# Where GpSimd waits for its scatters in a mixture-of-experts loop, and how its loop is closed

## The chip, the cores and the metric

The kernel runs on one core of a Trainium2 chip. The metric is the device time of one execution in microseconds (us): the median of the runs.

## The reference

A batch of 4 sequences of 768 tokens goes through a linear attention with decay (8 heads of 48), a dense layer pair 384 to 2048 to 384 with a leaky ReLU, and last a gated layer of 8 experts of which each token takes at most one. Only the last part bears on the change:

```
do_compute = x @ w_skip > 0
xc = x[do_compute]
logits = xc @ w_gate
e_idx = np.argmax(logits, axis=1)
for e in range(E):
    mask = e_idx == e
    h = np.maximum(xc[mask] @ w1[e], 0.0)
    y[mask] = gate_w[mask, None] * (h @ w2[e])
out[do_compute] = xc + y
```

The inputs are float32 and the result is a table of 3072 rows of 384 values.

## The kernel before

Attention and the dense layers are computed in eight groups of three chunks of 128 tokens. Each finished row z goes to DRAM twice, to a table `z_rows` and to `out`, while the routing of each chunk writes lists of token numbers by expert (`scatter`, line 1869). The expert part then works in blocks of up to 128 tokens of one expert. Two blocks of the busiest expert are done ahead of a loop, written out in full (names with `_a`, `AHEAD = 2`). All others are done in a loop over blocks whose number, `blocks`, is known only at run time (a value read from `plan`, at most 31). Each engine runs its own copy of the loop, `Fori(0, 8)` with four blocks written out in its body (`UNROLL = 4`) and an `If` on every turn and on every block. Every matmul is three products of high and low parts.

For block j of the loop:
- GpSimd (POOL) has gathered the block's rows of `z_rows` into `zg[u]`, u = j mod 4, with an indirect DMA (`gather`, line 1928).
- TensorE turns them (line 887), multiplies by w1 (line 964), turns the hidden rows (line 986) and multiplies by w2 into one of two banks (line 1003). ScalarE and VectorE make the high and low parts of what comes between (lines 1292 and 1820 for the hidden rows), and those of the next expert's weights.
- VectorE writes `res[j mod 2]` as bank times gate plus `zg[u]` (line 1844). It waits first for the product, `s_ey_done`, and for `s_res_free >= j + 1` (line 1843), which says that the buffer's last scatter has landed.
- GpSimd scatters `res[j mod 2]` to `out` with an indirect DMA (line 1962). Each such DMA adds 16 to `s_rows_out` when it has landed.

GpSimd's program around the loop sets the order of this. Before the loop it adds 1 to `s_res_free` (line 1935), gathers blocks 0 to 3 and scatters the two blocks done ahead (`scatter_ahead`, line 1903), which also count on `s_rows_out`. In `put_rows(j, ...)` it waits until all scatters before block j, those two included, have landed (line 1951) and adds 1 to `s_res_free`; copies the block's ids to `put` (line 1953); if there is a block j + 4, waits for the gather of block j and copies ids to `get` (line 1926); waits for `res` of block j; scatters it; and gathers block j + 4.

Its loop is in two levels: `part` of 0 and 1 (line 1970), each with an `If` whether that half has any block (line 1971), and in it four turns `jj` (line 1972) with an `If` of their own (line 1973). The other engines have one level of eight turns (VectorE: lines 1810 and 1811). After the loop GpSimd waits for all scatters (line 1978); then the block of engine programs closes with a branch, a DRAIN and a barrier on each engine (shown under line 100).

Of the kernel before, what the change touches and what calls it, by code (L numbers as in the profile page):

```python
# [42 lines left out]
TOKENS = B * S  # L43
# [4 lines left out]
BLOCKS = 31  # L48
# [4 lines left out]
UNROLL = 4  # L53
# [7 lines left out]
AHEAD = 2  # L61
# [31 lines left out]
def build(nc, rk_t, rk_nat, v_nat, w_cols, u_rows, win, wout, wout_t, gates, experts, consts, out, z_rows):  # L93
# [6 lines left out]
    with ctx:  # L100
# [3 lines left out]
        def sem(name):  # L104
            return ctx.enter_context(nc.semaphore(name))
# [93 lines left out]
        def sb4(name, shape, dt=F32):  # L199
            return sb(name, shape, dt, moe)  # L200
# [27 lines left out]
        id_put = sb4("id_put", [P, SPOTS], U32)  # L228
        sb4("gap2", [P, 100])
        res = [sb4(f"res{i}", [P, DM]) for i in range(2)]  # L230
# [13 lines left out]
        put = [sb4(f"put{i}", [P, 1], U32) for i in range(2)]  # L244
# [92 lines left out]
        rows_in = [sem(f"rows_in{i}") for i in range(UNROLL)]  # L337
        s_rows_out = sem("rows_out")
        s_res_free = sem("res_free")
# [9 lines left out]
        s_res_done = sem("res_done")  # L349
# [4 lines left out]
        s_ids_put = sem("ids_put")  # L354
# [13 lines left out]
        s_eht_a_lo = sem("eht_a_lo")  # L368
        s_ey_a_done = sem("ey_a_done")
        s_res_a = sem("res_a")  # L370
        s_spots = sem("spots")
        s_pool_past = sem("pool_past")
        s_dve_past = sem("dve_past")
# [271 lines left out]
        def _(pe):  # L645
# [332 lines left out]
            with pe.Fori(0, (BLOCKS + 1) // UNROLL) as jj:  # L978
                with pe.If(UNROLL * jj < blocks):
                    for u in range(UNROLL):  # L980
                        j = UNROLL * jj + u
                        with pe.If(j < blocks):
                            cur, odd, _, _, nxt, nxt_odd = entries(pe, regs, j)
                            pe.wait_ge(s_relu_done, j + 1)
                            for f in range(EFT):
                                mm = pe.transpose(eht_ps[f // 4][:, P * (f % 4):P * (f % 4) + P],  # L986
                                                  eh[:, P * f:P * f + P], ident)
                            mm.then_inc(s_eht_done, 1)

                            with pe.If(j < blocks - 1):  # L990
                                pe.wait_ge(s_zt_lo, j + 2)
                                pe.wait_ge(s_w1_lo, PIECES * nxt + PIECES)
                                first_product((u + 1) % 2, nxt_odd * EW)

                            with pe.If(j < blocks - 2):
                                pe.wait_ge(rows_in[(u + 2) % UNROLL], 16 * (jj + 1 + (u + 2) // UNROLL))
                                turn_rows((u + 2) % UNROLL)

                            pe.wait_ge(s_eht_lo, 2 * j + 2)
                            pe.wait_ge(s_w2_lo, PIECES * cur + PIECES)  # L1000
                            for f in range(EFT):
                                for a, b in ((eht_hi, w2_hi), (eht_hi, w2_lo), (eht_lo, w2_hi)):
                                    mm = pe.matmul(ey_ps[u % 2][:, 0:DM], a[:, f, :],  # L1003
                                                   b[:, bass.ds(odd * EW + DM * f, DM)],
                                                   start=f == 0 and a is eht_hi and b is w2_hi,
                                                   stop=f == EFT - 1 and a is eht_lo)
                            mm.then_inc(s_ey_done, 1)
# [842 lines left out]
        def _(pool):  # L1850
# [52 lines left out]
            def scatter_ahead(i):  # L1903
                pool.wait_ge(s_res_a, i + 1)
                pool.indirect_dma_start(
                    out=out[:, :], out_offset=bass.IndirectOffsetOnAxis(ap=put_a[:, i:i + 1], axis=0),
                    in_=zg_a[i][:], in_offset=None, bounds_check=TOKENS - 1,
                    oob_is_err=False).then_inc(s_rows_out, 16)

            for G in range(LATE):  # L1910
                scatter(G)
# [8 lines left out]
            def spot_at(reg, j):  # L1920

                pool.load(reg, plan[0:1, bass.ds(FIELDS * j + SPOT, 1)])
                return pool.snap(reg, min_val=0, max_val=SPOTS - 1)

            def pick_ids(u, spot_j):
                pool.tensor_copy(get[u][:], id_get[:, bass.ds(spot_j, 1)]).then_inc(s_ids_get, 1)

            def gather(u, j):
                pool.wait_ge(s_ids_get, j + 1)
                pool.sem_inc(s_pool_past, 1)  # L1930
                pool.indirect_dma_start(
                    out=zg[u][:], out_offset=None, in_=z_rows[:, :],
                    in_offset=bass.IndirectOffsetOnAxis(ap=get[u][:, 0:1], axis=0)).then_inc(rows_in[u], 16)

            pool.sem_inc(s_res_free, 1)
            pool.wait_ge(s_z_store, 16 * 2 * TILES)
            pool.wait_ge(s_plan_done, 1)
            blocks = pool.value_load(plan[0:1, TOTAL:TOTAL + 1], min_val=E, max_val=BLOCKS)
            reg = pool.alloc_register("pool_spot")
            far = pool.alloc_register("pool_far")  # L1940
# [6 lines left out]
            pool.wait_ge(s_spots, 2)  # L1947
            for i in range(AHEAD):
                scatter_ahead(i)
            def put_rows(j, u, turn):  # L1950
                pool.wait_ge(s_rows_out, 16 * (j + AHEAD))
                pool.sem_inc(s_res_free, 1)
                pool.tensor_copy(put[u % 2][:], id_put[:, bass.ds(spot_at(reg, j), 1)]).then_inc(s_ids_put, 1)
                pool.wait_ge(s_ids_put, j + 1)
                pool.sem_inc(s_pool_past, 1)
                with pool.If(j < blocks - UNROLL):
                    pool.wait_ge(rows_in[u], 16 * (turn + 1))
                    pool.sem_inc(s_pool_past, 1)
                    pick_ids(u, spot_at(far, j + UNROLL))
                pool.wait_ge(s_res_done, j + 1)  # L1960
                pool.sem_inc(s_pool_past, 1)
                pool.indirect_dma_start(
                    out=out[:, :], out_offset=bass.IndirectOffsetOnAxis(ap=put[u % 2][:, 0:1], axis=0),
                    in_=res[u % 2][:], in_offset=None, bounds_check=TOKENS - 1,
                    oob_is_err=False).then_inc(s_rows_out, 16)
                with pool.If(j < blocks - UNROLL):
                    gather(u, j + UNROLL)

            turns = (BLOCKS + 1) // UNROLL
            with pool.Fori(0, 2) as part:  # L1970
                with pool.If(turns // 2 * UNROLL * part < blocks):
                    with pool.Fori(0, turns // 2) as jj:
                        with pool.If(turns // 2 * UNROLL * part + UNROLL * jj < blocks):
                            for u in range(UNROLL):
                                j = turns // 2 * UNROLL * part + UNROLL * jj + u
                                with pool.If(j < blocks):
                                    put_rows(j, u, turns // 2 * part + jj)
            pool.wait_ge(s_rows_out, 16 * (blocks + AHEAD))


# ---- launch
# [47 lines left out]
```

## Time and profile before

| | us |
|---|---|
| runs | 677.17, 676.75, 675.28 |
| median | 676.75 |
| the profiled execution, whole | 677.17 |
| its span, first to last instruction | 675.4 |

| engine | busy us | share of the span |
|---|---|---|
| PE (TensorE matmul) | 648.7 | 96% |
| DVE (VectorE) | 401.9 | 60% |
| ACT (ScalarE) | 309.4 | 46% |
| POOL (GpSimd) | 83.6 | 12% |

A row of a view names line, engine, operation and the tiles written and read (out<-in). Names with a q at the end of the engine (POOLq, DVEq) are instructions of that engine's sequencer: waits, register operations, branches. They are not counted as busy time, but their starts are recorded, and they can be seen in the views of a line and of the chain.

### The profile page before, as it was taken

The numbers are of one execution on the slowest core, as the hardware profiler recorded it, in microseconds if no ns is written. First come the engines' busy times: TensorE is split into PE (matmuls) and PEld (weight loads), VectorE is DVE, ScalarE is ACT, GpSimd is POOL, SyncE is SP. The second block draws the span as 40 slices with busy tenths as digits, with TensorE's granted clock in tenths as the row PEclk, the third lists the DMA queues.
The fourth block names the chain that finished last, engine by engine and source line by source line (L and its number), as shares of the span: only waits on it lengthen the run. The fifth ranks groups of instructions, "written<-read, shape, count | busy, mean of one in ns | idle before, by whom it ended". The sixth has DMA issues, their size and how long they took to land.

```text
span 675.4 us, 14115 instructions
## 1 busy us (share of the span) xinstructions
PE 648.7 (96%) x4733; PEld 608.6 (90%) x4734; DVE 401.9 (60%) x864; ACT 309.4 (46%) x682; POOL 83.6 (12%) x102
## 2 busy tenths in 40 slices
PE   7889999999999999999999999999998989999993
PEld 6779889999999999999999999999998779999993
DVE  7876666645656575566556554743467644865851
ACT  5465534444344543444433445433355244855650
POOL 5140000100010001001000100010020131423311
PEclk9999999999999999999999999999999899999997
DMA  8936625220422222242104222003305277485300
GB/s 220 288 130 209 208 70 175 71 70 12 136 67 71 89 78 56 62 141 72 48 32 137 68 71 86 21 11 132 128 19 193 83 233 282 170 332 206 117 21 8
DMA packets 39324, 78.08 MB, mean 116 GB/s; under 512 B 9032, under 2 KB 27494, under 8 KB 39216
## 3 DMA queue, kind: packets, MB, share of 16 engines
q1 hardware_dynamic: 34272, 62.96, 29.6%
q10 hardware_dynamic: 2432, 9.76, 4.3%
q0 software_dynamic: 2560, 4.58, 2.2%
q8 instruction: 35, 0.57, 0.4%
q14 instruction: 25, 0.20, 0.1%
HBM read 61.68 MB, written 13.00 MB: 111 GB/s over the span
## 4 chain that ended last, share of the span: by engine, by line
PE 87%; DVE 4%; ACT 3%; DMA 3%; issue 2%; POOL 1%; SPq 0%; DVEq 0%; POOLq 0%; ACTq 0%
PE bank L797 30%; PE bank L817 29%; PE bank L1003 8%; PE bank L964 7%; PE bank L662 3%; PE bank L724 3%; DMA const<-in_consts 2%; PE bank L731 2%; PE bank L986 2%; PE bank L745 1%; PE bank L875 1%; ACT am L1072 1%; DMA rkt<-in_rk_t 1%; PE bank L851 1%; PE bank L887 1%
## 5 line engine op out<-in xcount | busy, mean ns | idle before, releaser
L1416 DVE TENSOR_TENSOR h_sb<-h_sb,bank 128x384 f32<-128x384 f32 x128 | 70.9, 554 | 158.3 <-ACT h_sb L1110 158.3
L1110 ACT ACTIVATE h_sb<-bank 128x384 f32<-128x384 f32 x128 | 62.9, 491 | 220.7 <-PE bank L797 220.6
L797 PE MATMUL bank<-x_hi,win_hi 128*128 128x384 f32 x384 | 135.0, 352 | 1.3 <-DVE win_lo L1461 0.9
L817 PE MATMUL bank<-wout_hi,g_hi 128*128 128x394 f32 x384 | 131.9, 343 | 1.5 <-DVE state L1392 1.5
L817 PE MATMUL bank<-wout_hi,g_lo 128*128 128x394 f32 x384 | 131.2, 342 | 0.0
L817 PE MATMUL bank<-wout_lo,g_hi 128*128 128x394 f32 x384 | 131.1, 341 | 0.0
L797 PE MATMUL bank<-x_hi,win_lo 128*128 128x384 f32 x384 | 129.4, 337 | 0.0
L797 PE MATMUL bank<-x_lo,win_hi 128*128 128x384 f32 x384 | 129.2, 336 | 0.0
L1423 DVE TENSOR_TENSOR g_lo<-h_sb,g_hi 128x384 fp32r<-128x384 f32 x128 | 71.7, 560 | 30.9 <-ACT g_hi L1117 29.9
L1117 ACT ACTIVATE g_hi<-h_sb 128x384 fp32r<-128x384 f32 x128 | 66.8, 522 | 49.2 <-DVE h_sb L1416 48.0
L1876 POOL DMA_INDIRECT id_list<-idgate,dst x24 | 24.4, 1015 | 453.1 <-DVE dst L1612 448.3
L797 PEld LDWEIGHTS bank<-x_hi,win_hi 128*128 128x128 f32 x384 | 72.1, 188 | 8.6 <-issue 6.1
L817 PEld LDWEIGHTS bank<-wout_hi,g_hi 128*128 128x128 f32 x384 | 72.2, 188 | 1.8 <-issue 1.8
L817 PEld LDWEIGHTS bank<-wout_lo,g_hi 128*128 128x128 f32 x384 | 72.3, 188 | 0.0
L817 PEld LDWEIGHTS bank<-wout_hi,g_lo 128*128 128x128 f32 x384 | 72.3, 188 | 0.0
L797 PEld LDWEIGHTS bank<-x_lo,win_hi 128*128 128x128 f32 x384 | 72.3, 188 | 0.0
L797 PEld LDWEIGHTS bank<-x_hi,win_lo 128*128 128x128 f32 x384 | 72.1, 188 | 0.0
L1072 ACT ACTIVATE am<-const,diag 128x128 f32<-128x128 f32 x184 | 58.2, 392 | 3.3 <-DVE diag L1365 3.2
L1003 PE MATMUL bank<-w_hi,eht_hi 128*128 x96 | 33.9, 353 | 2.2 <-DVE eht_lo L1820 2.2
L1003 PE MATMUL bank<-w_hi,eht_lo 128*128 x96 | 32.8, 342 | 0.0
L1003 PE MATMUL bank<-w_lo,eht_hi 128*128 x96 | 32.8, 342 | 0.0
L1379 DVE COPY_PREDICATED am<-const,bank 128x512 f32<-128x512 uint32 x46 | 31.2, 731 | 0.4 <-ACT am L1072 0.4
(244 smaller groups left out, 894.9 us busy)
## 6 DMA issues: line engine op xcount, KB each, us to landing
raw<-in_experts SPq DMA_DIRECT2D x32, 768.0 KB, 5.8
rkt<-in_rk_t SPq DMA_DIRECT2D x46, 192.0 KB, 3.7
rkn<-in_rk_nat SPq DMA_DIRECT2D x21, 384.0 KB, 4.1
v<-in_v_nat SPq DMA_DIRECT2D x24, 192.0 KB, 2.9
z_rows<-z_sb SPq DMA_DIRECT2D x24, 192.0 KB, 2.8
out<-z_sb SPq DMA_DIRECT2D x24, 192.0 KB, 2.8
stage<-in_win ACTq DMA_DIRECT2D x4, 768.0 KB, 4.9
stage<-in_wout_t ACTq DMA_DIRECT2D x4, 768.0 KB, 7.6
```

The lines of the kernel that those rows point to most:

```text
L662: mm = pe.matmul(scores_in(n)[q][:, P * p:P * p + P], kb[n % 2][rows, p, :], rt[n % 2][rows, p, :], start=True, stop=True)
L797: mm = pe.matmul(h_ps[t % 2][:, 0:GT], a[:, kk, cols], b[G % 2][:, kk, :], start=n == 0, stop=n == 3 * KT - 1)
L817: mm = pe.matmul(z_ps[i][:, 0:ZW], a[t % 3][:, tok], b[:, f, :], start=f == 0 and j == 0, stop=f == FT - 1 and j == 2)
L964: mm = pe.matmul(eh_ps[c][:], a[par][:, kk, :], b[:, bass.ds(base + EF * kk + 512 * c, 512)], start=kk == 0 and a is zt_hi and b is w1_hi, ...
L1003: mm = pe.matmul(ey_ps[u % 2][:, 0:DM], a[:, f, :], b[:, bass.ds(odd * EW + DM * f, DM)], start=f == 0 and a is eht_hi and b is w2_hi, sto ...
L1072: ins = act.activation(am_of(n)[h % 2][:, h // 2, :], ident, ACT.Copy, scale=diag_of(n)[:, h:h + 1])
L1110: act.activation(h_sb[t % 2][:], h_ps[t % 2][:, 0:GT], ACT.Copy, scale=SLOPE).then_inc(s_h_scaled, 1)
L1117: act.activation(g_hi[t % 3][:], h_sb[t % 2][:], ACT.Copy).then_inc(s_g_hi_done, 1)
L1379: dve.copy_predicated(am_of(n)[q][:], spread(before.bitcast(U32), 1, [P, PAIRS, P]), scores_in(n)[q][:].rearrange("a (p t) -> a p t", p=PA ...
L1416: dve.tensor_tensor(h_sb[t % 2][:], h_sb[t % 2][:], h_ps[t % 2][:, 0:GT], ALU.max).then_inc(s_leaky, 1)
L1423: dve.tensor_tensor(g_lo[t % 3][:], h_sb[t % 2][:], g_hi[t % 3][:].bitcast(F32), ALU.subtract).then_inc(s_g_lo_done, 1)
L1876: pool.indirect_dma_start(out=id_list[:, :], out_offset=bass.IndirectOffsetOnAxis(ap=dst[:, n:n + 1], axis=0), in_=idgate[:, n, :], in_off ...
```

## The change

GpSimd's program is changed, and nothing else. The two scatters ahead count on a semaphore of their own, `s_rows_a_out`, that is waited for only after the loop. `s_res_free` starts with 2. In the loop, blocks with u of 1 to 3 still wait first for all earlier scatters of the loop; a block with u = 0 doesn't, and a block with u = 3 waits instead, at its end, for its own scatter and all before it, and adds to `s_res_free` there. The two levels of the loop become one with eight turns.

```diff
+        s_rows_a_out = sem("rows_a_out")
...
-                    oob_is_err=False).then_inc(s_rows_out, 16)
+                    oob_is_err=False).then_inc(s_rows_a_out, 16)
...
-            pool.sem_inc(s_res_free, 1)
+            pool.sem_inc(s_res_free, 2)
...
-            def put_rows(j, u, turn):
-                pool.wait_ge(s_rows_out, 16 * (j + AHEAD))
-                pool.sem_inc(s_res_free, 1)
-                pool.tensor_copy(put[u % 2][:], id_put[:, bass.ds(spot_at(reg, j), 1)]).then_inc(s_ids_put, 1)
...
-            turns = (BLOCKS + 1) // UNROLL
-            with pool.Fori(0, 2) as part:
-                with pool.If(turns // 2 * UNROLL * part < blocks):
-                    with pool.Fori(0, turns // 2) as jj:
-                        with pool.If(turns // 2 * UNROLL * part + UNROLL * jj < blocks):
-                            for u in range(UNROLL):
-                                j = turns // 2 * UNROLL * part + UNROLL * jj + u
-                                with pool.If(j < blocks):
-                                    put_rows(j, u, turns // 2 * part + jj)
-            pool.wait_ge(s_rows_out, 16 * (blocks + AHEAD))
+            with pool.Fori(0, (BLOCKS + 1) // UNROLL) as jj:
+                with pool.If(UNROLL * jj < blocks):
+                    for u in range(UNROLL):
+                        j = UNROLL * jj + u
+                        with pool.If(j < blocks):
+                            if u > 0:
+                                pool.wait_ge(s_rows_out, 16 * j)
+                                pool.sem_inc(s_res_free, 1)
+                            pool.tensor_copy(put[u % 2][:], id_put[:, bass.ds(spot_at(reg, j), 1)]).then_inc(s_ids_put, 1)
...
+                            pool.wait_ge(s_res_done, j + 1)
+                            pool.sem_inc(s_pool_past, 1)
+                            pool.indirect_dma_start(
+                                out=out[:, :], out_offset=bass.IndirectOffsetOnAxis(ap=put[u % 2][:, 0:1], axis=0),
+                                in_=res[u % 2][:], in_offset=None, bounds_check=TOKENS - 1,
+                                oob_is_err=False).then_inc(s_rows_out, 16)
+                            with pool.If(j < blocks - UNROLL):
+                                gather(u, j + UNROLL)
+                            if u == UNROLL - 1:
+                                pool.wait_ge(s_rows_out, 16 * (j + 1))
+                                pool.sem_inc(s_res_free, 1)
+            pool.wait_ge(s_rows_out, 16 * blocks)
+            pool.wait_ge(s_rows_a_out, 16 * AHEAD)
```

## Rows read from the trace of the kernel before

**Rows 1.** The page's chain that ended last, by engine.
```profile
PE 87%; DVE 4%; ACT 3%; DMA 3%; issue 2%; POOL 1%; SPq 0%; DVEq 0%; POOLq 0%; ACTq 0%
```

**Rows 2.** The chain from 615 us on: start us, us, what.
```profile
634.65 4.19 PE bank L1003 x24
638.84 0.87 PE bank L986 x8
639.71 4.12 PE bank L964 x18
643.83 0.33 PE bank L887 x3
...
666.71 0.63 DVE res L1844
...
667.36 0.02 POOLq L1961
...
667.44 0.03 POOLq L1962
...
668.26 0.93 POOL out L1962
```

**Rows 3.** The scatters' line: count, first and last start, time to landing.
```profile
L1962 POOL DMA_INDIRECT out<-res,put x12: 980/1010/1019, 564.4 to 668.2; - x12
...
DMA to landing us min/median/max: 2.2/3.5/6.3
```

**Rows 4.** DMA queues, 655 to 676 us: packets, MB, share of 16 engines.
```profile
q0 software_dynamic: 128, 0.14, 1.9%
```

**Rows 5.** Line 100 (the end): duration ns min/median/max, first and last start.
```profile
L100 POOLq EVENT_SEMAPHORE  x2: 17/17/17, 675.2 to 675.3; - x2
...
L100 DVEq DRAIN  x1: 17/17/17, 670.6 to 670.6; - x1
L100 POOLq COMPARE_BRANCH  x1: 43/43/43, 670.7 to 670.7; - x1
L100 POOLq DRAIN  x1: 4324/4324/4324, 670.9 to 670.9; - x1
```

**Rows 6.** The closing branches of the loops, 667 to 676 us, and line 1978.
```profile
L1972 POOLq COMPARE_BRANCH  x2: 48/50/53, 668.2 to 668.9; - x2
...
L1970 POOLq COMPARE_BRANCH  x2: 40/46/53, 669.0 to 669.7; - x2
...
L1978 POOLq FUSED_REGOPS  x1: 48/48/48, 669.7 to 669.7; - x1
...
L1810 DVEq COMPARE_BRANCH  x5: 50/56/56, 667.6 to 670.5; - x5
```

**Rows 7.** The program's first line: GpSimd's DRAIN at the start.
```profile
L2020 POOLq DRAIN  x1: 188/188/188, 0.4 to 0.4; - x1
```

**Rows 8.** Waits, 538 to 676 us: who, for whom, us in total, times, longest.
```profile
DVE res L1844 <- PE bank L1003: 18.9, 6, 6.3
...
POOL put L1953 <- DMA out<-zg_a,put_a: 7.8, 1, 7.8
...
POOL out L1962 <- POOL get L1926: 1.4, 2, 0.7
```

**Rows 9.** Lines 1952 and 1843 in 555 to 562 us.
```profile
L1952 POOLq EVENT_SEMAPHORE  x1: 17/17/17, 557.0 to 557.0; - x1
...
L1843 DVEq EVENT_SEMAPHORE  x1: 21/21/21, 559.9 to 559.9; - x1
```

**Rows 10.** Timelines of POOL and of PE: block 4's scatter, block 8's gather and turning.
```profile
603.50 1.01 POOL L1962 DMA_INDIRECT out<-res,put  x1 [0.70 <-POOL get L1926]
604.82 0.98 POOL L1931 DMA_INDIRECT zg<-z_rows,get  x1 [0.30 <-issue]
...
624.63 0.49 PE L887 MATMUL bank<-const,zg 128*128 128x128 f32 x3
```

More of the change, by code:

```diff
@@ L1949, in _ @@
                 scatter_ahead(i)
-            def put_rows(j, u, turn):
-                pool.wait_ge(s_rows_out, 16 * (j + AHEAD))
-                pool.sem_inc(s_res_free, 1)
-                pool.tensor_copy(put[u % 2][:], id_put[:, bass.ds(spot_at(reg, j), 1)]).then_inc(s_ids_put, 1)
[L1954 to L1967, printed above, removed]
@@ L1978, in _ @@
-            pool.wait_ge(s_rows_out, 16 * (blocks + AHEAD))
+            with pool.Fori(0, (BLOCKS + 1) // UNROLL) as jj:
[7 more added lines that the diff above has]
+                            pool.tensor_copy(put[u % 2][:], id_put[:, bass.ds(spot_at(reg, j), 1)]).then_inc(s_ids_put, 1)
+                            pool.wait_ge(s_ids_put, j + 1)
+                            pool.sem_inc(s_pool_past, 1)
+                            with pool.If(j < blocks - UNROLL):
+                                pool.wait_ge(rows_in[u], 16 * (jj + 1))
+                                pool.sem_inc(s_pool_past, 1)
+                                pick_ids(u, spot_at(far, j + UNROLL))
+                            pool.wait_ge(s_res_done, j + 1)
+                            pool.sem_inc(s_pool_past, 1)
+                            pool.indirect_dma_start(
+                                out=out[:, :], out_offset=bass.IndirectOffsetOnAxis(ap=put[u % 2][:, 0:1], axis=0),
+                                in_=res[u % 2][:], in_offset=None, bounds_check=TOKENS - 1,
+                                oob_is_err=False).then_inc(s_rows_out, 16)
+                            with pool.If(j < blocks - UNROLL):
+                                gather(u, j + UNROLL)
+                            if u == UNROLL - 1:
+                                pool.wait_ge(s_rows_out, 16 * (j + 1))
+                                pool.sem_inc(s_res_free, 1)
```

## The prediction

> **What bounds the kernel now.** I read the chain of waits first. It is TensorE's for 87% of the span and GpSimd's for 1% [rows 1], and in the expert loop it repeats one pattern without a gap: 4.19 + 0.87 + 4.12 + 0.33 = 9.51 us a block, all of it matmuls [rows 2]. So a change on GpSimd pays or costs inside the loop only if it makes TensorE wait. It is different at the two ends. The reader should look at what comes after the last matmul: the last `res` from 666.71 for 0.63, two sequencer steps, and the last scatter's issue at 668.2 [rows 2, 3]. The chain view stops there, so the rest comes from the views of single lines. The closing branch of GpSimd's program runs at 670.7, its DRAIN takes 4.324 us from 670.9, and only then, at 675.2, do its barrier's semaphores go out and the program ends [rows 5]. What held the branch at 670.7 is the scatter's landing: the shortest time to landing is 2.2 us and the median 3.5 [rows 3], and 668.2 + 2.5 = 670.7. GpSimd had done its own bookkeeping before that, the last loop branch at 669.7 and the register step of the final wait at 669.7 [rows 6]. That is 1.0 us early. This order, loop first and landing last, is what the change turns round.
>
> **How many turns are empty.** The scatter line has 12 instructions [rows 3], so `blocks` is 12: three full turns of four, and block 11, the last, has u = 3. Eight turns less three are five empty ones. VectorE already has this form, one loop of eight: its closing branch runs 5 times from 667.6 to 670.5 [rows 6], 2.9 us for four steps, 0.73 us per empty turn. GpSimd's two levels run only one empty inner turn and skip the second half: the inner closing branches stand at 668.2 and 668.9, 0.7 apart, the outer ones at 669.0 and 669.7, 0.7 apart as printed (0.6 to 0.8 with the rounding) [rows 6].
>
> **The change at the end of the program.** Removed from the end: one empty turn and one skipped half, which lay under the scatter's flight and are worth nothing. Added: in block 11 GpSimd waits for the landing of its own scatter *before* it leaves the body. Queued behind that wait are the increment, the back edge, the five empty turns, the two final waits, the branch and the DRAIN, and for the DRAIN's end all engines wait. Step by step from the landing at 670.7:
> - the increment of `s_res_free`: one semaphore instruction. L1961 starts at 667.36 and the next step at 667.44 [rows 2], so 0.08.
> - the back edge of turn 2: a register step and the branch. By the spacing of neighbouring sequencer steps, two at 0.08 or a little under: 0.15.
> - five empty turns. Bounds: 0.6 from below (outer branches, the least that rounding allows), 0.73 from above (VectorE). The new loop has the outer loop's simple form, without the sum over `part`. I take 0.64, near the lower end: 5 x 0.64 = 3.2 (3.0 to 3.65).
> - the final wait is now two, each found satisfied: one more semaphore step, 0.08, and a register step that used to lie under the flight, 0.05.
>
> The sum is 0.08 + 0.15 + 3.2 + 0.13 = 3.56, rounded 3.5, with bounds 3.3 and 4.0. The closing branch moves from 670.7 to 674.2. If the DRAIN costs what it costs now, the end moves by the same 3.5 us. Here is the one term that the trace doesn't settle: the price of a DRAIN that begins later. Its bounds are 4.32 as now (nothing hidden) and 4.32 - 3.5 = 0.8 (its end is fixed by something set off at the scatter, and all of the addition lies under it). GpSimd's other DRAIN, at the program's start and behind no DMA, takes 0.188 [rows 7], so the DRAIN does depend on what went before. Against a fixed end: no packet of any queue but the scatters' own 128 moves in the last 21 us [rows 4], and those of the last scatter have landed when the DRAIN begins. I take 4.32, as work that the DRAIN itself does.
>
> The other engines' DRAINs are short: VectorE's takes 17 ns [rows 5]. The Trainium skill ("VectorE: DVE Perf Modes", The DRAIN you can't avoid) says that the DRAINs of pre- and postamble are about 12 ns, constant, on all five engines. The VectorE row is near that and GpSimd's is 4324 ns, so for GpSimd the trace disagrees; whoever holds to the rule must take those 4.3 us for a wait on something and not for the DRAIN's own cost, which is rival B below.
>
> On the price of a turn, the branches last 40 to 56 ns as recorded [rows 6], yet a turn takes 0.7. The Trainium skill ("Advanced Engine Details and Errata", Control Flow Timing) gives about 108 ns for a compare-and-branch. An estimate by that page, with two branches a turn and nothing else, is 5 x 0.216 = 1.1 us in place of 3.2; the measured spacing decides, since it holds the whole turn.
>
> **The change at the start of the loop.** `s_res_free` begins at 2 and block 0 no longer waits for the two scatters ahead. That wait is the 7.8 us of GpSimd in the waits [rows 8]. Who gains? The semaphore step after it, which releases block 1's `res`, runs at 557.0; VectorE reaches its own wait of block 0 only at 559.9 [rows 9] and then waits for TensorE's product anyway (six such waits, 18.9 us) [rows 8]. Even block 0's first release was there from the start. So the gain is 0. The cover is 2.9 us plus a whole block: were it gone, each us of a later landing would cost a us in `res`, and TensorE would notice only after that. The two id copies of block 0 move about 8 us earlier, on an engine that then waits for `res`. The new final wait for the scatters ahead comes over 100 us after they land: 0 beyond its step, counted above.
>
> **The change inside the loop.** At blocks 1, 2, 3 and their like nothing moves. The wait between u = 3 and u = 0 is the same wait for the same landing, but the back edge and the two `If`s, once under the flight, now come behind it: one turn's branching, 0.6 to 0.7 us, at the two boundaries 3 to 4 and 7 to 8. Queued behind it on GpSimd are the copies of ids, the scatter of block 4 and the gather of block 8. At the first boundary GpSimd is already late: block 4's scatter waited for its own ids, not for `res` [rows 8, 10], so it comes about 0.7 later, at 604.2, and the gather at 605.5 instead of 604.82. TensorE turns those rows at 624.63 [rows 10]. Even with 6.3 us to landing [rows 3], 12 us are left. Cost 0; with that cover gone it would be twice 0.7, 1.4 us, and I keep no more of it than the rivals below. `res_free` itself is given right at the landing, as early as before.
>
> **The sum.** The profiled execution took 677.17, 1.8 above its span. 677.17 + 3.5 = 680.7 for it. It is 0.42 above the median of the runs; on the median, 676.75 + 3.5 = 680.25, say 680.3.
>
> **Rivals.**
> B. *The DRAIN hides the empty turns.* If its end is fixed from the last scatter (issued 668.2, DRAIN ends 675.2, 7.0 us later), the DRAIN begins later and is shorter: 676.8, no change, and between 676.8 and 680.3 if a part is fixed. For it: 188 ns at the start against 4324 at the end. Against: nothing in the trace is in flight.
> C. *The start of the loop gains, and more than the end loses.* It is the wait for the scatters ahead that could hold VectorE's `res`, from the point where they land later than 559.9, 2.9 us later than here. In this execution its price is 0. Were the landing 6 us later it would bring some 3 us back; with both the end's cost and this, about 676.8 + 3.5 - 6 = 674 at the best. Only executions unlike the one profiled would show it.
> D. *Each empty turn costs more.* A taken branch over the whole body could stall. The one empty inner turn (0.7) and VectorE's five (0.73) show no stall. If each turn cost 1.5, the sum would be 7.5 + 0.36, and the time 684.6. The Trainium skill ("Runtime: NRT & Kernel Launch", Instruction fetch mechanics) says that a taken branch to outside a window of two pages makes the sequencer fetch by DMA first. The last 21 us show no packet of an instruction queue [rows 4], with five jumps on VectorE in them.
>
> **Chances.** Forecast (end later by 3.3 to 4.0): 0.77. B: 0.13. C: 0.03. D: 0.07. About 0.3%, 2.0 us, is what a measurement of this kernel can tell from no change. The forecast and D are slower, B is mostly no change. Faster 0.03, same 0.14, slower 0.83. The forecast's own range is 679.3 to 681.3, its bounds and the spread of runs, which is 1.9 us here. Left alone it leaves out too much, so the range reaches down over B, to 676.3, and up to 681.5.
>
> **What would show it.** In the changed kernel's profile: GpSimd's loop branch runs five times after the last landing, 0.6 to 0.73 apart; its closing branch is near 674.2; the DRAIN after it lasts 4.3. TensorE's pattern keeps 9.5 us a block, and block 0's ids are copied by 550. A DRAIN of about 1 us would make B right and this wrong; turns of over 1 us, D; a last matmul well before 666.6, C.

## The result and the profile after

In interleaved runs the changed kernel took 679.33 us (median of 12) and the kernel before 674.99 us (median of 12). The ratio is 1.006, with a 95% interval of 1.004 to 1.0081: 4.1 us slower, between 2.7 and 5.5. A second comparison, told below, gave 1.0058 (1.0039 to 1.0076), 3.9 us. The forecast was 3.5 us slower, to 680.3 us.

The profiled execution of the changed kernel took 678.46 us with a span of 676.6, only 1.3 us and 1.2 us over the profiled one of before. The span alone would mislead: the two executions differ by 2.3 us before the loop writes its first `res`. The row of that line in the changed kernel (duration ns min/median/max, first and last start) goes from 560.6 to 664.5; before it went from 562.9 to 666.7. From the first to the last `res` that is 103.9 us against 103.8: the loop is as long as before.

```profile
L1845 DVE SCALAR_TENSOR_TENSOR res<-bank,found,zg x12: 610/614/618, 560.6 to 664.5; 128x384 f32<-128x384 f32 x12
```

TensorE's granted clock makes most of those 2.3 us, and it differs from execution to execution. At about 521 us TensorE stands idle for 2.05 us in all twelve traces of this study. Behind that the clock was at 0.5 (1.2 GHz) for 3.4 us in seven of them, the one of before included, and at 1.0 (2.4 GHz) throughout in five, the changed kernel's included. From the first gather of the blocks done ahead to the first `res` it is 57.9 to 58.0 us in the seven and 56.4 in the five, 1.6 less. The same happens in the last block of the loop, where TensorE stands idle for 2.21 us until VectorE has written the low part of the hidden rows: the clock then fell to 0.5 for some 3 us in ten traces, before and changed among them, and the last `res` came 8.6 to 8.7 us behind the one ahead of it, but in e2_one_level and e4_more_turns it stayed at 1.0 and `res` came after 7.1. Two rows show it (window, its length, TensorE's busy us, granted clock, share and rate of DMA), the first of the changed kernel, the second of e2_one_level:

```profile
659.00:661.00 2.00, 2.00 (x8) 0.50 0.02 4
```
```profile
659.00:661.00 2.00, 2.00 (x12) 1.00 0.06 17
```

So I compare the *tail*: from the start of the last scatter to the end of the span. Before it was 668.2 [rows 2, 3] to the span's 675.4, 7.2 us. In the changed kernel it is 666.0 to 676.6, 10.6 us, 3.4 more. The chain of waits of the changed kernel (start us, us, what) keeps the pattern of [rows 2] up to that scatter; the lines have moved by one, and the scatter's by six:

```profile
632.36 4.19 PE bank L1004 x24
636.55 0.87 PE bank L987 x8
637.42 4.12 PE bank L965 x18
641.54 0.33 PE bank L888 x3
...
664.49 0.63 DVE res L1845
...
666.00 0.98 POOL out L1968
```

What lies behind it is seen in the views of single lines of the changed kernel, of 667 us on (the fences' columns are those of [rows 5]). First the wait that the change put at the end of block 11, line 1976, and then the loop's own line 1951 and the `If` of its turns, line 1952:

```profile
L1976 POOLq EVENT_SEMAPHORE  x1: 17/17/17, 668.5 to 668.5; - x1
```
```profile
L1951 POOLq ALU_OP  x6: 32/32/36, 668.6 to 671.6; - x6
L1951 POOLq COMPARE_BRANCH  x6: 48/53/53, 668.6 to 671.7; - x6
L1951 POOLq FUSED_REGOPS  x5: 35/35/41, 668.9 to 671.4; - x5
```
```profile
L1952 POOLq COMPARE_BRANCH  x5: 45/45/45, 669.0 to 671.4; - x5
```

The landing releases line 1976 at 668.5, 2.5 behind the scatter's start as before. The back edge follows at 668.6, and then five empty turns: six closing branches from 668.6 to 671.7, 0.61 us apart. Before, there were four such rows in their place, two of the inner loop and two of the outer; the last was at 669.7, ahead of the landing [rows 6]. The end of the program, line 100:

```profile
L100 POOLq EVENT_SEMAPHORE  x2: 17/17/17, 676.5 to 676.5; - x2
...
L100 DVEq DRAIN  x1: 17/17/17, 668.4 to 668.4; - x1
...
L100 POOLq COMPARE_BRANCH  x1: 38/38/38, 671.9 to 671.9; - x1
L100 POOLq DRAIN  x1: 4322/4322/4322, 672.1 to 672.1; - x1
```

The closing branch now comes 5.9 us behind the scatter's start in place of 2.5, and the DRAIN takes 4.322 in place of 4.324 [rows 5]: nothing of the delay went under it, though it began 3.4 us later behind the scatter's start.

### The profile page after: what moved, and what is told of

Same layout as the page of the kernel before. It is cut to its first block, busy times and chain, and to the rows that moved or that the text cites. A ratio compares the mean times of both kernels' runs of the same rounds, so it can differ in the third digit from the quotient of the medians.

```text
span 676.6 us, 14123 instructions
## 1 busy us (share of the span) xinstructions
PE 648.1 (96%) x4733; PEld 608.4 (90%) x4734; DVE 401.7 (59%) x864; ACT 309.6 (46%) x682; POOL 80.2 (12%) x102
## 4 chain that ended last, share of the span: by engine, by line
PE 87%; DVE 4%; ACT 3%; DMA 2%; issue 2%; POOL 1%; SPq 0%; DVEq 0%; ACTq 0%; POOLq 0%
PE bank L798 30%; PE bank L818 28%; PE bank L1004 8%; PE bank L965 7%; PE bank L663 3%; PE bank L725 3%; PE bank L732 2%; DMA const<-in_consts 2%; PE bank L987 2%; PE bank L746 1%; PE bank L876 1%; ACT am L1073 1%; PE bank L888 1%; DMA rkt<-in_rk_t 1%; DVE w_lo L1508 1%
```

## The experiments

Every kernel was timed against the kernel before on the same chip. The tail comes from one profile of each. The columns give us from the start of the last scatter to GpSimd's closing branch (or, where the last wait is gone or a DRAIN follows it, to the DRAIN), the length of the closing DRAIN, and the tail.

| kernel | last scatter | closing branch or DRAIN behind it | closing DRAIN | tail | ratio to before (95%) |
|---|---|---|---|---|---|
| before | 668.2 | 2.5 | 4.32 | 7.2 | |
| changed | 666.0 | 5.9 | 4.32 | 10.6 | 1.0060 (1.0040 to 1.0081) |
| e1_two_levels | 666.2 | 4.3 | 4.32 | 9.0 | 1.0031 (1.0016 to 1.0046) |
| e2_one_level | 665.0 | 3.2 | 4.32 | 7.9 | 1.0007 (0.9983 to 1.0031) |
| e3_own_sem | 666.0 | 2.5 | 4.32 | 7.2 | 1.0009 (0.9987 to 1.0030) |
| e4_more_turns | 666.5 | 7.7 | 4.32 | 12.4 | 1.0093 (1.0064 to 1.0121) |
| e5_sync_waits | 666.2 | 1.5 | 4.32 | 6.1 | 0.9988 (0.9967 to 1.0009) |
| e6_drains | 667.7 | 2.6 | 1.70 + 0.05 | 4.6 | 0.9960 (0.9939 to 0.9982) |
| e8_loop_drains | 667.4 | 2.5 | 0.13 | 3.0 | 0.9935 (0.9911 to 0.9959) |
| e7_early_end | 665.8 | 1.5 | 1.05 | 2.8 | 0.9903 (0.9880 to 0.9926) |
| e9_after_drains | 666.5 | 5.9 | 0.12 | 6.4 | 0.9980 (0.9962 to 0.9999) |
| e10_after_again | 666.2 | 5.9 | 4.32 | 10.6 | 1.0058 (1.0039 to 1.0076) |

### The waits of the changed kernel, the loop of before

```diff
-            with pool.Fori(0, (BLOCKS + 1) // UNROLL) as jj:
-                with pool.If(UNROLL * jj < blocks):
+            with pool.Fori(0, 2) as part:
+                with pool.If(turns // 2 * UNROLL * part < blocks):
+                    with pool.Fori(0, turns // 2) as jj:
+                        with pool.If(turns // 2 * UNROLL * part + UNROLL * jj < blocks):
```

> The changed kernel with its waits and semaphores, but GpSimd's loop again in two levels of 2 and 4 turns, so that one empty inner turn and one skipped outer half follow the last landing in place of five empty turns. I call tail what lies between the start of the last scatter and the end of the span: 7.2 us before (668.2 to 675.4), 10.6 after (666.0 to 676.6). Theory (the cost is what GpSimd's sequencer does behind the landing, at some 0.6 to 0.7 us a turn): 1.8 us behind the landing instead of 3.5, tail 9.0, time 1.8 us over before. Rival (the wait at the end of block 3 and its like costs, not the turns): tail 10.6 as after and time 3.5 to 4.3 over before.

The end of this kernel, line 100:

```profile
L100 POOLq COMPARE_BRANCH  x1: 38/38/38, 670.5 to 670.5; - x1
L100 POOLq DRAIN  x1: 4324/4324/4324, 670.7 to 670.7; - x1
```

The last scatter's row there starts at 666.24, so the branch is 4.3 behind it, where 2.5 + 1.8 was expected. The tail is 9.0 as the theory had it, and the time 2.1 us over before (1.1 to 3.1). The moved wait by itself, with one empty turn and one skipped half behind it, costs 1.8; the other 1.6 of the 3.4 are turns that the one-level loop adds.

### The loop of the changed kernel, the waits of before

```diff
-            with pool.Fori(0, 2) as part:
-                with pool.If(turns // 2 * UNROLL * part < blocks):
...
+            with pool.Fori(0, (BLOCKS + 1) // UNROLL) as jj:
+                with pool.If(UNROLL * jj < blocks):
+                    for u in range(UNROLL):
+                        j = UNROLL * jj + u
+                        with pool.If(j < blocks):
+                            put_rows(j, u, jj)
```

> The kernel before with its waits at the head of each block, but GpSimd's loop as one level of eight turns. The five empty turns start right behind the last scatter's issue and take 3.1 us; the landing takes 2.5 us. Theory: 0.7 to 0.8 us show, closing branch 3.2 us behind the scatter's start in place of 2.5, tail 8.0, time 0.8 over before, which this measurement can hardly tell from nothing. Rival (turns cost by themselves wherever they stand): tail 10.6, time 3.5 or more over before.

The `If` of its turns, line 1970, from 664 us on, and its line 100:

```profile
L1970 POOLq COMPARE_BRANCH  x5: 45/45/45, 665.4 to 667.8; - x5
```
```profile
L100 POOLq COMPARE_BRANCH  x1: 38/38/38, 668.3 to 668.3; - x1
```

The `If` of the first empty turn runs 0.3 us behind the scatter's start (665.03), and the closing branch comes at 3.2, not at the landing's 2.5. The tail is 7.9, and the time is not told apart from before (0.5 us over, -1.1 to 2.1), as expected. Alone the loop costs 0.75 and the wait 1.8; together 3.4, more than the sum of 2.6, since each takes the other's cover away: the wait lets the turns begin only at the landing.

### The start of the change alone

```diff
-                    oob_is_err=False).then_inc(s_rows_out, 16)
+                    oob_is_err=False).then_inc(s_rows_a_out, 16)
...
-            pool.sem_inc(s_res_free, 1)
+            pool.sem_inc(s_res_free, 2)
...
-                pool.wait_ge(s_rows_out, 16 * (j + AHEAD))
-                pool.sem_inc(s_res_free, 1)
+                if u > 0:
+                    pool.wait_ge(s_rows_out, 16 * j)
+                    pool.sem_inc(s_res_free, 1)
+                else:
+                    with pool.If(turn > 0):
+                        pool.wait_ge(s_rows_out, 16 * j)
+                        pool.sem_inc(s_res_free, 1)
```

> The kernel before with the start of the change alone: the two scatters ahead count on their own semaphore, res_free starts at 2, block 0 does not wait for them; the loop keeps two levels and its waits stay at the head of each block (for u = 0 behind an If on the turn). Theory: VectorE's and TensorE's times in the loop stay as before (9.5 us a block), tail 7.2, time within 0.3% of before. Rival (the start gains by freeing GpSimd 8 us earlier, which would have hidden a part of the loss in the changed kernel): 1 us or more faster than before.

Timeline of GpSimd in this kernel (start us, us, what, idle before it and what ended it):

```profile
546.59 1.00 POOL L1906 DMA_INDIRECT out<-zg_a,put_a  x1 [0.30 <-issue]
547.74 0.18 POOL L1959 COPY put<-id_put 128x1 uint32 x1
548.90 0.18 POOL L1927 COPY get<-id_get 128x1 uint32 x1 [0.98 <-issue]
562.15 0.99 POOL L1968 DMA_INDIRECT out<-res,put  x1 [13.06 <-DVE res L1845]
```

The 7.8 us of waiting for the scatters ahead [rows 8] are gone, and GpSimd waits 13.06 for `res` instead. The time is 0.6 us over before (-0.9 to 2.0) and the tail 7.2. The start brings nothing that can be seen.

### Eight more turns behind the last wait

```diff
             pool.wait_ge(s_rows_out, 16 * blocks)
+            pool.sem_inc(s_pool_past, 1)
+            with pool.Fori(0, 8) as kk:
+                with pool.If(UNROLL * kk + BLOCKS < blocks):
+                    pool.sem_inc(s_pool_past, 1)
```

> The changed kernel with eight more empty turns of a loop behind the last wait for the loop's scatters, with an If that never holds, and a body of one instruction only. Theory: each turn costs 0.6 us, so 4.9 to 5.3 us more with the loop's start, tail 15.7 to 16.0, the DRAIN 4.32 again; time 5 us over the changed kernel, 8.5 to 9.5 over before. If a turn's price is that of the jump over a long body, the short turns take 0.3 to 0.4 and the tail is 13.5. Rival (the DRAIN ends at a fixed time behind the last DMA, once the 7 us are over it shrinks): the DRAIN shorter than 4.3 and the tail less by as much.

The added loop's line in this kernel:

```profile
L1979 POOLq ALU_OP  x8: 32/32/35, 672.5 to 674.1; - x8
L1979 POOLq COMPARE_BRANCH  x8: 40/45/53, 672.6 to 674.1; - x8
```

The size was missed. The trace has no row for the `If`, which can never hold and so seems to have been left out of the program: a turn is one register step and one taken branch, 0.21 us. In the trace's starts, the next row follows the taken branch of this short loop 0.16 us later, and that of the long loop (line 1951) 0.25 to 0.26 later. That points to a dearer jump over the long body, but the next instruction is of another kind in the two, so it is not shown. The order holds: eight such turns add 1.8 to the tail (12.4), the time is 6.3 us over before (4.3 to 8.2), and the DRAIN, which now begins 7.8 us behind the last scatter, still takes 4.322. That rules out an end fixed by the last DMA.

### The last wait on SyncE

```diff
+            sp.wait_ge(s_plan_done, 1)
+            blocks = sp.value_load(plan[0:1, TOTAL:TOTAL + 1], min_val=E, max_val=BLOCKS)
+            sp.wait_ge(s_rows_out, 16 * (blocks + AHEAD))
+            sp.sem_inc(s_w1_in, 1)
...
-            pool.wait_ge(s_rows_out, 16 * (blocks + AHEAD))
```

> The kernel before, but the last wait for all scatters stands at the end of SyncE's program and not of GpSimd's. GpSimd's closing branch follows its loop at once, 1.6 us behind the last scatter's start, and its DRAIN begins before the landing. Theory (the DRAIN costs a fixed 4.32 us of its own): it ends 0.9 us earlier, tail 6.3, time 0.9 under before. Rival (the DRAIN's end is tied to the last DMA's landing or issue): DRAIN longer, tail 7.2, time as before.

Line 100 of it:

```profile
L100 POOLq DRAIN  x1: 4322/4322/4322, 667.8 to 667.8; - x1
L100 SPq DRAIN  x1: 7/7/7, 668.8 to 668.8; - x1
```

GpSimd's DRAIN begins 1.5 behind the scatter (666.24), ahead of the landing (SyncE, which waits for it, reaches its own DRAIN at 668.8), and takes the same 4.322. The tail is 6.1; the time is 0.8 under before with an interval that holds zero (-2.2 to 0.6) and the tail's gain of 1.1 as well, so the gain is shown in the tail alone.

### Two more DRAINs

```diff
                 scatter_ahead(i)
+            pool.drain()
...
             pool.wait_ge(s_rows_out, 16 * (blocks + AHEAD))
+            pool.sem_inc(s_pool_past, 1)
+            pool.drain()
```

> The kernel before with two more DRAINs on GpSimd: one in front of its loop, right behind the issue of the two scatters ahead, where it waits for their landing anyway, and one behind the last wait, just before the closing one. Theory A (each DRAIN behind DMAs costs 4.3 whatever went before): the one in front of the loop takes 4.3 and is hidden, both at the end take 4.3, tail 11.6. Theory B (the first DRAIN clears what the DMAs left, the next is short): 4.3 or more for the first, about 0.2 for the last, tail 7.5; the one in front of the loop is then 4.3 or, if the price grows with the DMAs issued, 28 of them there against 48 at the end, shorter than 4.3.

The added DRAINs, lines 1950 and 1981, and the closing one:

```profile
L1950 POOLq DRAIN  x1: 9543/9543/9543, 547.9 to 547.9; - x1
```
```profile
L1981 POOLq DRAIN  x1: 1700/1700/1700, 670.3 to 670.3; - x1
```
```profile
L100 POOLq DRAIN  x1: 46/46/46, 672.0 to 672.0; - x1
```

Neither theory had 1.70, and the count of DMAs in the expectation was off: up to the first added DRAIN GpSimd has issued 24 + 2 + 4 + 2 = 32 indirect DMAs, and behind it 8 gathers and 12 scatters, 20 of 52 in all. 1.70 / 20 = 0.085 and 4.32 / 52 = 0.083. So a DRAIN seemed to work off each indirect DMA issued since the last one, and the next two kernels were made to test that. The first added DRAIN, with DMAs in flight, took 9.5, though 32 of them would be 2.7; it lay where GpSimd had to wait anyway. The kernel was 2.7 us faster than before (1.2 to 4.1).

### A DRAIN in every block

```diff
+                pool.drain()
                 pool.wait_ge(s_res_done, j + 1)
```

> The kernel before with one more DRAIN on GpSimd in every block of its loop, behind the copies of ids and ahead of the wait for res, where GpSimd is idle. Theory (a DRAIN works off the indirect DMAs issued since the last one, some 0.083 us each: 4.32 for 52, 1.70 for 20 in the kernel with two more DRAINs): the first one in the loop takes 2.7 us for 32, those of blocks 1 to 8 about 0.17 for two, 9 to 11 about 0.08 for one, the closing one 0.1; TensorE keeps 9.5 us a block; tail 7.2 - 4.2 = 3.0 us, time 4.2 us under before. Rival (the price goes by the time since the last DRAIN, or by the bytes moved): the DRAINs of blocks 9 to 11 are not shorter than those of 1 to 8. Rival (a DRAIN in the loop waits for gathers in flight and delays the scatter): TensorE's pattern gets longer than 9.5 us and the time is not under before.

The added line's DRAINs, in three answers for three stretches (block 0, block 1, the last three blocks), and the closing one:

```profile
L1960 POOLq DRAIN  x1: 2907/2907/2907, 557.7 to 557.7; - x1
```
```profile
L1960 POOLq DRAIN  x1: 448/448/448, 570.8 to 570.8; - x1
```
```profile
L1960 POOLq DRAIN  x3: 116/118/132, 644.0 to 662.2; - x3
```
```profile
L100 POOLq DRAIN  x1: 126/126/126, 670.1 to 670.1; - x1
```

2.91 for 32 DMAs, 0.22 to 0.45 in seven of the eight blocks with two (1.48 in block 7, not explained), 0.12 to 0.13 for one, also at the end. Most pairs cost at least twice what was expected. The one of 1.48 begins at 625.69, 0.2 behind the landing of the last gather at 625.49, so nothing was in flight. The price falls with the count and not with the time since the last DRAIN: blocks 9 to 11 come about as far apart as the others. Nor does it go by bytes: 24 of the 32 DMAs ahead of the first DRAIN are the list scatters of the routing, whose rows are 8 bytes against 1536, and the 32 still cost 0.09 each, where the 20 of e6_drains, all of long rows, cost 0.085. TensorE keeps its pattern (4.19 at 633.79, the next at 643.30, 9.51 apart; first to last `res` 103.9 us), the tail is 3.0, and the time is 4.4 us under before (2.8 to 6.0).

### The same, with the last wait on SyncE

The edit is that of e8_loop_drains and that of e5_sync_waits together.

> The same DRAIN in every block, and the last wait for all scatters at the end of SyncE's program and not of GpSimd's. Theory: GpSimd's closing DRAIN begins 1.5 us behind the last scatter's start with one DMA to work off; if it needs that DMA's landing it ends at 2.6, if not at 1.7; the landing itself, at 2.5, then holds SyncE, so the tail is 2.7 to 2.9 either way, 0.1 to 0.3 under the kernel with the DRAINs alone, and the time 4.3 us under before. Rival (the closing DRAIN has a base price that only a late start shows): tail 3.5 or more.

Line 100 of it:

```profile
L100 POOLq DRAIN  x1: 1053/1053/1053, 667.3 to 667.3; - x1
L100 DVEq DRAIN  x1: 17/17/17, 668.2 to 668.2; - x1
L100 SPq DRAIN  x1: 7/7/7, 668.4 to 668.4; - x1
```

The closing DRAIN has one DMA left, begins 1.0 ahead of its landing and ends with it, at 668.35, as SyncE's does. So a DRAIN does wait for what is in flight. The tail is 2.8, 0.2 less than with the DRAINs alone; the time is 6.5 us under before (5.0 to 8.1, from six runs). The tail explains 4.4 of it; the rest, which the interval does not take away, was not traced to a cause. (Its trace is one of the five without the clock's fall at 521 us; whether its six runs had fewer such falls than those of before is not on record.) This kernel has the lowest ratio of the study and is faster than both the kernel before and the changed one; from e8_loop_drains, whose interval overlaps, it is not told apart.

### DRAINs in the changed kernel, and the changed kernel again

The first is the changed kernel with `pool.drain()` ahead of its wait for `res_done`; the second is the changed kernel as it stands.

> The changed kernel with a DRAIN in every block as in the kernel before with loop drains. Theory (the empty turns behind the landing and the DRAIN are two terms in series): the closing branch stays 5.9 us behind the last scatter's start, the closing DRAIN is 0.13, tail 10.6 - 4.2 = 6.4, time 0.8 under before. Rival (the late closing hides or shares a part with the DRAIN): tail below 6.0 or above 6.9.

> The changed kernel again, to see whether the 4.3 us of the first comparison hold or whether they are the 3.4 that its tail shows. Theory: 3.4 over before, tail 10.6. Rival (something ahead of the last scatter also costs, about 0.9 us): 4.3 over before again, with the last scatter's start later than before's in the profile.

Line 100 of the first, and its DRAIN in block 6:

```profile
L100 POOLq COMPARE_BRANCH  x1: 38/38/38, 672.4 to 672.4; - x1
L100 POOLq DRAIN  x1: 116/116/116, 672.6 to 672.6; - x1
```
```profile
L1966 POOLq DRAIN  x1: 3377/3377/3377, 617.3 to 617.3; - x1
```

The branch stays 5.9 behind the scatter (666.50) and the tail is 6.4: the turns behind the landing and the DRAIN are two terms in series. The time is 1.3 us under before (0.1 to 2.6). The DRAIN of block 6 took 3.4, to 620.7, with a gather of 614.19 in flight that landed at 620.6; it still cost TensorE nothing: the `res` of the blocks around it come 9.04, 9.52 and 10.6 us apart, as in the changed kernel. This kernel's first DRAIN in the loop, in block 0 at 549.25, took 7.2 us, since the wait for the scatters ahead no longer stands in front of it, and ended 1.4 behind their last landing at 555.05; `res` came only at 561.1, so that cost nothing either. The changed kernel again is 3.9 us over before (2.6 to 5.1), tail 10.6. Both comparisons hold the 3.4 of the tail; neither gives ground for a second cost ahead of the last scatter, and by their intervals, which reach 5.5 and 5.1, neither excludes one of up to some 2 us. In the traces the loop itself leaves no room for it (first to last `res` 103.8 us before, 103.9 in both of the changed kernel).

## Why the prediction was right

The mechanism came as forecast: turns that used to lie under the last flight now follow the landing, and the closing DRAIN follows them at its old price. The time itself was helped by luck. The forecast of 680.3 was 3.5 on top of 676.75, the median of three runs; over twelve runs the kernel before takes 674.99. So the starting point was 1.8 us too high and the step by the two medians 0.8 too small (4.3 against 3.5), and the two errors cancel in part: 679.33 is 0.9 under the forecast. One reading was wrong without harm: the pattern is not "without a gap", since TensorE idles 2.21 us in the last block, and `res` comes 8.0 to 10.6 us apart and not every 9.51; all of it is the same in both kernels.

**Empty turns.** Five, as counted from 12 blocks and u = 3 of the last. The price taken was 0.64 us, measured 0.61: 3.06 in place of 3.2.

**The steps around them.** Increment and back edge 0.08 and 0.15 against 668.5 to 668.6; from the last loop branch at 671.7 to the closing branch at 671.9. All of it with the turns is 3.44 (5.93 less 2.48), against the sum of 3.56, which was set down as 3.5. The two single changes show that neither makes the cost alone.

**The DRAIN.** The price was taken as 4.32 wherever it begins, and so it was: 4.322 to 4.324 in every kernel without added DRAINs, beginning from 1.5 to 7.8 us behind the last scatter's start. Rival B is out. The reason given, work that the DRAIN itself does, is borne out and has a size now, some 0.083 us for each indirect DMA issued since the last DRAIN. That nothing was in flight told against an end fixed elsewhere, but was no reason for a fixed price.

**The start of the loop.** Gain 0, by the kernel with that part alone. The copies of block 0 run at 547.55 and VectorE's line 1844 at 557.6, which waits for TensorE afterwards. In the changed kernel GpSimd's timeline reads:

```profile
547.55 0.22 POOL L1959 COPY put<-id_put 128x1 uint32 x1
548.76 0.18 POOL L1927 COPY get<-id_get 128x1 uint32 x1 [0.99 <-POOL put L1959]
562.12 0.99 POOL L1968 DMA_INDIRECT out<-res,put  x1 [13.18 <-DVE res L1845]
```

**The boundary between turns.** Block 4's scatter was to come 0.7 later against its `res`. It does: 601.89 is 2.77 behind the `res` of 599.12, where before the scatter at 603.50 [rows 10] was 2.09 behind a `res` of 601.41. The gather goes out at 603.21, and TensorE turns those rows at 622.34, 19 us later.

```profile
601.89 1.01 POOL L1968 DMA_INDIRECT out<-res,put  x1 [0.69 <-POOL get L1927]
603.21 0.98 POOL L1932 DMA_INDIRECT zg<-z_rows,get  x1 [0.30 <-issue]
```

**Rivals C and D.** C needed a `res` that waits for the scatters ahead; none did. The sign that was named for it, a last matmul well before 666.6, did come, at 664.3, but it is no sign of C: the execution was 2.3 ahead at its first `res`, of which the clock makes 1.6, and the traces of e5_sync_waits and e7_early_end, which keep the wait for the scatters ahead, have that first `res` at 560.9 and 560.4, where the changed kernel's two have 560.6 and 560.8. C's sum was off too: by its own working a landing 6 us later brings 3 back and not 6, so that the changed kernel would end at some 677 and gain nothing. D's price of over 1 us a turn is excluded by 0.61, and the changed kernel, too, moves no packet of an instruction queue from 655 us on. The measured ratio gives 4.1 us where the steps give 3.4; the difference is inside the interval.

## What to carry to other kernels

A wait for a DMA should be the last thing that an engine does, and loop turns that do nothing belong ahead of it: here the same five turns cost 0.75 us under a flight of 2.5 us and 3.1 behind it. At the end of a program, look beyond the chain of waits at the sequencers' rows of the closing line, for a DRAIN that all engines wait for. On GpSimd its price can be paid early, with a DRAIN in stretches where that engine is idle; here that took 4.2 us off the tail, where the change had added 3.4.

## What the runs showed of the hardware that was not expected

GpSimd's DRAIN works off the indirect DMAs issued since its last one: 4.32 us for 52, 2.91 for 32, 1.70 for 20, 0.12 to 0.13 for one, 0.046 for none. For two that had landed it took 0.22 to 0.57, but 1.48 in block 7 of e8_loop_drains and of e7_early_end, which is not explained; so the count gives the size for many and not the exact price of a few. It waits for the landing of those in flight: the closing one of e7_early_end, begun 1.0 ahead of the landing, and three in the loops of e7_early_end and e9_after_drains end 0.1 behind it, and it took 9.5 with the scatters ahead and the gathers in flight. The work on those that have landed goes on meanwhile: the DRAIN that began 1.0 us ahead of the last landing with 52 to work off took 4.322, no longer than one that began behind it. What the work is was not tried, nor whether plain DMAs count the same. The Trainium skill ("VectorE: DVE Perf Modes", The DRAIN you can't avoid) has closing DRAINs at about 12 ns on all engines; here ScalarE's took 8 ns, SyncE's 7 and VectorE's 17. TensorE's (of the sequencer that loads weights) took 8 in six traces and 210 to 263 in the other six, the changed kernel's 255 among them, not explained and waited for by nobody, since GpSimd's ends last. On GpSimd the 12 ns do not hold: 4322 to 4324 behind 52 DMAs, and 46 with none since the last DRAIN.

An empty turn of GpSimd's loop, with an `If` and two taken branches, costs 0.61 us, one with a single taken branch 0.21, though the branch rows themselves last 0.04 to 0.05.
